# Attention and two MLPs on one core: auxiliary rows behind the next head's load, the last head ahead of the sums, additions on GpSimd moved, x divided in place

## What is computed

```python
def _attn_ref(q, k, v, s):                       # 4 batches x 8 heads, 576 tokens, 64 wide
    scores = scale * np.matmul(q, k.transpose(0, 1, 3, 2))
    cum = np.cumsum(np.maximum(s, 0.0), axis=-1)
    bias = -(cum[:, :, :, None] - cum[:, :, None, :])
    scores = np.where(causal, -1000000000.0, scores + np.minimum(bias, 0.0))
    attn = np.exp(scores - np.max(scores, axis=-1, keepdims=True))
    attn = attn / (np.sum(attn, axis=-1, keepdims=True) + 1e-09)
    return np.matmul(attn, v)

def _moe_ref(x, w_in, w_out, g_ln):              # 2304 tokens, 512 -> 1024 -> 512
    h = x @ w_in
    e = np.exp(h - np.max(h, axis=-1, keepdims=True))
    solu = h * (e / (np.sum(e, axis=-1, keepdims=True) + 1e-09))
    ln = (solu - mean(solu)) / np.sqrt(var(solu) + 1e-06) * g_ln
    return ln @ w_out

def _moe2_ref(x, w1, w2, w3, w_out):             # 512 -> 768 -> 512
    return np.maximum(np.maximum(x @ w1, x @ w2), x @ w3) @ w_out
```

## Time and profile before

| what | value |
|---|---|
| median of three runs | 773.01 us (772.12, 773.01, 778.3) |
| the profiled execution | 773.02 us, span 771.2 us |
| TensorE matmuls | 722.3 us busy, 94% of the span |
| VectorE | 394.9 us, 51% |
| ScalarE | 327.0 us, 42% |
| GpSimd | 251.4 us, 33% |
| DMA | 59.42 MB, mean 77 GB/s |

### The profile page before, as it was taken

How to read it: one execution, slowest core, us unless ns; L and a number is a source line. 1 busy time by engine, 2 the same in 40 slices (tenths; PEclk the granted TensorE clock), 3 DMA queues, 4 the chain that set the end, 5 groups by cost and what they waited for, 6 DMA issues and landing times.

```text
span 771.2 us, 12703 instructions
## 1 busy us (share of the span) xinstructions
PE 722.3 (94%) x4248; PEld 664.4 (86%) x4248; DVE 394.9 (51%) x702; ACT 327.0 (42%) x795; POOL 251.4 (33%) x248
## 2 busy tenths in 40 slices
PE   2799999999878899999999999999999999999997
PEld 2788888888767688989898989999989999899995
DVE  8898988888853675636354364612203213132120
ACT  1798888898853443424233242412112112121111
POOL 6766779888872842606040200000000000000000
PEclk9999999999998999999999999999999999999999
DMA  6598887878765312306100031000010000100101
GB/s 142 114 215 195 198 184 181 186 185 190 160 146 113 84 35 48 82 1 170 36 0 0 0 106 59 1 14 28 1 42 1 13 29 1 38 2 0 41 0 41
DMA packets 58227, 59.42 MB, mean 77 GB/s; under 512 B 23572, under 2 KB 45204, under 8 KB 58164
## 3 DMA queue, kind: packets, MB, share of 16 engines
q1 hardware_dynamic: 58196, 59.02, 32.0%
HBM read 44.15 MB, written 10.10 MB: 70 GB/s over the span
## 4 chain that ended last, share of the span: by engine, by line
PE 71%; DVE 8%; issue 6%; POOL 5%; DMA 4%; ACT 3%; SPq 2%; DVEq 0%; POOLq 0%; ACTq 0%
PE ps L652 10%; PE ps L653 10%; PE ps L651 10%; PE ps L584 4%; PE ps L586 4%; PE ps L585 4%; DMA qk_raw<-in_qk_dram 4%; PE ps L572 3%; PE ps L574 3%; PE ps L573 3%; PE ps L664 3%; PE ps L665 3%; PE ps L666 3%; PE ps L481 3%; DVE lnT_lo L1170 1%
## 5 line engine op out<-in xcount | busy, mean ns | idle before, releaser
L653 PE MATMUL ps<-x_lo,w_hi 128*128 (+1 forms) x432 | 144.4, 334 | 0.0
L651 PE MATMUL ps<-x_hi,w_hi 128*128 128x384 f32 x432 | 144.4, 334 | 0.0
L652 PE MATMUL ps<-x_hi,w_lo 128*128 128x384 f32 x432 | 144.4, 334 | 0.0
L481 PE MATMUL ps<-ident,probs 128*128 128x128 f32 x480 | 78.2, 289 | 21.9 <-DVE pt_lo L1069 15.6
L844 ACT ACTIVATE probs<-ps,nmax 128x576 f32<-128x576 f32 (+4 forms) x160 | 83.0, 539 | 17.7 <-DVE nmax L1062 17.5
L1069 DVE TENSOR_TENSOR pt_lo<-ps,pt_hi 128x512 fp32r<-128x512 f32 (+1 forms) x128 | 78.3, 652 | 11.6 <-ACT pt_hi L854 8.3
L481 PEld LDWEIGHTS ps<-ident,probs 128*128 128x128 f32 x480 | 52.4, 144 | 33.9 <-DVE pt_lo L1069 21.7
L651 PEld LDWEIGHTS ps<-x_hi,w_hi 128*128 128x128 f32 x432 | 81.1, 188 | 0.2
L652 PEld LDWEIGHTS ps<-x_hi,w_lo 128*128 128x128 f32 x432 | 81.1, 188 | 0.2
L653 PEld LDWEIGHTS ps<-x_lo,w_hi 128*128 128x128 f32 x432 | 81.1, 188 | 0.0
L854 ACT ACTIVATE pt_hi<-ps 128x512 fp32r<-128x512 f32 (+1 forms) x128 | 69.9, 572 | 26.4 <-PE ps L481 22.6
(11 more groups left out here) (101 smaller groups left out, 1436.3 us busy)
## 6 DMA issues: line engine op xcount, KB each, us to landing
qk_raw<-in_qk_dram SPq DMA_DIRECT2D x64, 288.0 KB, 4.4
xT<-halves SPq DMA_DIRECT2D x32, 144.0 KB, 2.5
xb_dram<-halves SPq DMA_DIRECT2D x32, 144.0 KB, 2.4
xb<-xb_dram SPq DMA_DIRECT2D x24, 192.0 KB, 3.9
rinvB<-rsum_dram SPq DMA_DIRECT2D x24, 192.0 KB, 4.1
stage<-in_moe_w_dram SPq DMA_DIRECT2D x18, 256.0 KB, 4.3
out_dram<-stage SPq DMA_DIRECT2D x18, 256.0 KB, 2.0
v_raw<-in_v_dram SPq DMA_DIRECT2D x32, 128.0 KB, 4.1
```

Source lines behind the costliest of these rows:

```text
L481: mm = pe.transpose(ps[:, GBANK[g], P * n:P * (n + 1)], probs[1 - par][:, o:o + P], ident[:, :])
L651: pe.matmul(dst, w_hi[f][:, i, c, :], x2_hi[par][:, c, :], start=(c == 0), stop=False)
L652: pe.matmul(dst, w_lo[f][:, i, c, :], x2_hi[par][:, c, :], start=False, stop=False)
L653: mm = pe.matmul(dst, w_hi[f][:, i, c, :], x2_lo[:, c, bass.ds(g * GT, GT)], start=False, stop=(c == KC - 1))
```

## The change

1. `reload(t)` loads q and k of head t, the values of head t-2, and then the auxiliary rows of head t-1 (not t), for which it waits for the scores of head t-3.
2. Head 31 is loaded before `store_rinv`. Its auxiliary rows come behind `store_rinv`, and the loads and stores behind these have another order.
3. On GpSimd `join(0)` goes behind the split of head 31 and of head 29's values, and `divide(0)` directly behind it, ahead of the split of head 30's values. `join(1)` stays between the values of heads 30 and 31.
4. `rinvB` has two buffers, and `divide` writes into `xT`; `xg` is gone. `divide(g)` no longer waits for `x_lo_ready`. `load_rinv(g)` is issued one group earlier.

```diff
+            def reload_aux(t, par):
+                sp.wait_ge(scores_done, 3 * (t - 1))
+                load_aux(t, par)
...
                 load_qk(t, par)
                 if known is None or known >= 4:
                     reload_v(t - 2, par)
-                if known == 2:
+                if known == 3:
                     sp.wait_ge(aux_stored, 16)
-                sp.wait_ge(scores_done, 3 * (t - 1))
-                load_aux(t, par)
+                if known is None or known >= 3:
+                    reload_aux(t - 1, 1 - par)
                 if known is None or known >= 5:
                     store_x(t - 5, 1 - par)
...
             reload(HEADS - 2, 0)
+            reload(HEADS - 1, 1)
             sp.wait_ge(rinv_done, 1)
             store_rinv(slice(0, LAST))
-            reload(HEADS - 1, 1)
+            reload_aux(HEADS - 1, 1)
+            reload_v(HEADS - 2, 0)
+            store_x(HEADS - 5, 1)
             sp.wait_ge(rinv_stored, 16 * NCH)
             load_rinv(0)
-            load_xb(1)
-            reload_v(HEADS - 2, 0)
-            store_x(HEADS - 5, 1)
             reload_v(HEADS - 1, 1)
             store_x(HEADS - 4, 0)
+            load_rinv(1)
+            load_xb(1)
             store_x(HEADS - 3, 1)
+            store_x(HEADS - 2, 0)
             load_xb(2)
             sp.wait_ge(xg_ready, 1)
-            load_rinv(1)
-            store_x(HEADS - 2, 0)
+            load_rinv(2)
             store_x(HEADS - 1, 1)
...
-            for g in range(2, NG):
-                sp.wait_ge(xg_ready, g)
+            for g in range(3, NG):
+                load_xb(g)
+                sp.wait_ge(xg_ready, g - 1)
                 load_rinv(g)
-                if g + 1 < NG:
-                    load_xb(g + 1)
...
-            def divide(g, known):
+            def divide(g, par):
                 cols = xT[:, :, bass.ds(g * GT, GT)]
-                pool.wait_ge(rinvB_loaded, 64 * (g + 1))
-                if known != 0:
-                    pool.wait_ge(x_lo_ready, 3 * g)
+                pool.wait_ge(rinvB_loaded[par], (g - par) * 32 + 64)
                 pool.wait_ge(x_added, g + 1)
-                pool.tensor_tensor(xg[:, :, :], cols, rinvB[:, :, :], ALU.mult).then_inc(xg_ready, 1)
+                pool.tensor_tensor(cols, cols, rinvB[par][:, :, :], ALU.mult).then_inc(xg_ready, 1)
...
+            slot(HEADS - 2, 0, HEADS - 2)
             join(0)
-            slot(HEADS - 2, 0, HEADS - 2)
+            divide(0, 0)
             slot(HEADS - 1, 1, HEADS - 1)
             join(1)
-            divide(0, 0)
             slot(HEADS, 0, HEADS)
-            divide(1, None)
+            divide(1, 1)
             join(2)
```

More of the change, by code:

```diff
@@ L111, in attention_and_mlp @@
         ab_.__enter__()
-        rinvB = sb(ab_, "rinvB", [P, KC, GT])
-        xg = sb(ab_, "xg", [P, KC, GT])
+        rinvB = [sb(ab_, f"rinvB{i}", [P, KC, GT]) for i in range(2)]
         xb = sb(ab_, "xb", [P, KC, GT])
@@ L220, in attention_and_mlp @@
         wout_lo_ready = sem("wout_lo_ready")
-        rinvB_loaded = sem("rinvB_loaded")
+        rinvB_loaded = [sem(f"rinvB_loaded{i}") for i in range(2)]
         xg_ready = sem("xg_ready")
@@ L393, in load_rinv @@
                         src = rsum_dram[HB * b_:HB * (b_ + 1), s0:s0 + GT // 2].rearrange("(j r) t -> r j t", r=2)[par:par + 1]
-                        dst = rinvB[D * par:D * (par + 1), :, part * GT // 2:(part + 1) * GT // 2]
-                        sp.dma_start(dst, src.broadcast_to([D, KC, GT // 2])).then_inc(rinvB_loaded, 16)
+                        dst = rinvB[g % 2][D * par:D * (par + 1), :, part * GT // 2:(part + 1) * GT // 2]
+                        sp.dma_start(dst, src.broadcast_to([D, KC, GT // 2])).then_inc(rinvB_loaded[g % 2], 16)
             LAST = HEADS - HB
@@ L811, in group @@
                 if more and not first:
-                    divide(g + 1, None)
+                    divide(g + 1, 1 - base)
                 for i in range(3):
@@ L911, in x_high @@
                     act.wait_ge(h_done, 3 * g + i - 1)
-                act.activation(x_hi[ab][:, :, :], xg[:, :, P * i:P * (i + 1)], ACT.Copy).then_inc(x_hi_ready, 1)
+                act.activation(x_hi[ab][:, :, :], xT[:, :, bass.ds(g * GT + P * i, P)], ACT.Copy).then_inc(x_hi_ready, 1)
             def gate(g, i, ab, first):
@@ L1122, in x_low @@
                 dve.wait_ge(x_hi_ready, 3 * g + i + 1)
-                dve.tensor_tensor(x_lo[ab][:, :, :], xg[:, :, P * i:P * (i + 1)], f32(x_hi[ab][:, :, :]),
+                dve.tensor_tensor(x_lo[ab][:, :, :], xT[:, :, bass.ds(g * GT + P * i, P)], f32(x_hi[ab][:, :, :]),
                                   ALU.subtract).then_inc(x_lo_ready, 1)
```

## The result

The changed kernel takes 767.65 us (median of 7 runs, 766.3 to 770.56) beside 773.47 us (7 runs) of the kernel before on the same chip: a ratio of 0.9925, with an interval of 0.9897 to 0.9952. That is 5.8 us less, where 12.6 were forecast (760.4, range 756 to 767). The kernel is faster, but by less than 1%, and lies 0.65 us outside the range. The profiled execution took 766.3 us, with a span of 764.5 us; that of before had 771.2, so the two traces differ by 6.7 us.

What follows compares the result with a forecast made beforehand. TensorE was taken as the bound, so only its waits and slow clock could give time back. Terms 3.4 + 0.9 + 4.2 + 3.6 + 0.5 = 12.6 us took 773.0 to 760.4 us, range 756 to 767.

Steps and rivals of the forecast that it cites:

- Part 1: Slots 3 to 27: auxiliary rows behind the next head's load let qk_raw come earlier; 3.4 us net of charges.
- one of the two places named: SP's next stop after L301: the store of the outputs (x_copied) or the split of the previous head; no separate size.
- 4.5 - 0.5: Slots 3 to 26: 4.5 us from earlier loads, less 0.5 for PE waiting on later auxiliary rows.
- the 0.5 charged: Slots other than 27: cost of auxiliary rows landing late for PE, 0.5 us; slot 27 had its own 0.6.
- the 5.6 us: Slots 3 to 26: their excess over undisturbed slots of 6.21 us, taken as the upper bound of the gain.
- Part 2: Slots 28 and 30: earlier loads, with join(0) later on GpSimd, win 0.9 us and 4.2 us.
- Part 3: Slot 32 to the first hidden matmul: GpSimd's reordered additions and divisions win 3.6 us; in-place division 0.
- The clock's term: First hidden matmul and its neighbours: 0.5 us added because they no longer run at the low clock.
- A: Early slots and slot 28 gain nothing because DMA engines keep loads late: 764.7; 0.21 jointly with the GpSimd rival.
- B: Seam: divide(0) or join(1) delays a split_v 2 us beyond cover, clock falls: 764.4; 0.21 jointly with the DMA rival.
- the forecast's own case: Whole kernel: the expected outcome, 757.5 to 762.5 us, given a chance of 0.56.

Runs made afterwards that it cites:

- all three versions: Versions where divide(2) has no wait for x_low: the changed kernel, 767.65 us; the kernel before with in-place division, 782.66; the fastest version without the wait, 766.05.

## Why the prediction was right and wrong

**Part 1, the auxiliary rows.** Right in its mechanism, 1.0 us too high. SP waits at L300 no more; it waits for the copied outputs (L341, 29.2 us in 23 pieces), one of the two places named. Slots 3 to 26 gained 3.0 us, where 4.5 - 0.5 were put. The waits for the rows in them were 0.46, 0.17 and 0.49, 1.1 against the 0.5 charged, but the slots with them (6, 8 and 10) are together only 0.4 us over the normal 6.21 each. More is left where the prediction put nothing: slots 17, 21 and 25 still wait 0.35 us each for `pt_lo` and take 6.68 us, 1.4 too much together. So 4.5 of the 5.6 us was too much to expect. Slot 27 waited 1.11 us and became 0.5 longer, against 0.6.

The Trainium skill, DMA: Bandwidth & Descriptors, Queues, rings and completion order, was cited for the small load not landing ahead of the `v` load. The two versions with the order turned round are consistent with it: with `v` issued first PE waited 0.17 to 0.49 us in early slots, with the rows first not at all. They don't prove it, since the rows are then also issued about 1.2 us earlier. And in slot 27 the `v` loads were not what counted: with the rows ahead of them the wait was still 1.03 us.

**Part 2, slots 28 and 30.** Right: 1.0 for 0.9, and 4.25 for 4.2. The two runs that take one half away show that, with the rest of the change, neither half does it alone.

**Part 3, the seam.** Right in size (3.7 for 3.6), and in that GpSimd blocks no `v_hl`: PE has no wait for it. The path was somewhat other. GpSimd's rows there:

```profile
216.58 3.49 POOL L781 TENSOR_TENSOR xT<-xT,rinvB 128x1536 f32<-128x1536 f32 x1 [1.94 <-DMA rinvB<-rsum_dram]
...
225.88 3.50 POOL L774 TENSOR_TENSOR xT<-xT,xb 128x1536 f32<-128x1536 f32 x1 [4.99 <-DMA xb<-xb_dram]
```

`divide(0)` waited 1.94 us for `rinvB` and ended at 220.07, 2.9 us earlier than the 223.0 worked out, as all of the seam stands 2.9 us earlier than put there (slot 31 starts at 214.58, not 217.45: the prediction held slots 3 to 26 unchanged on that scale). Relative to slot 31 it ends 5.5 us after its start, as forecast.

**The step that failed** is the last of Part 3: "Dividing in place removes no instruction; it lets `divide(g+1)` go before `x_low` has read the old tile. PE doesn't wait for `xg` after 250 us, so it is worth 0, with bounds of 1 us either way for VectorE's and GpSimd's shared use of memory." Its first half is true. But it asked only who waits for the division, and not what the division runs beside once nothing holds it back. It measures a loss of 5.5 us (5.6 to 6.3 in the stage) against 0 with bounds of 1. Rows of before for such a collision were there and not used (they are shown above): `wout_lo` with a longest of 1535 ns against a median of 742 and `normalize` with 2.94 us, where it takes 1.20 elsewhere. They show that the two engines delay each other: there it is 0.8 us of delay under an instruction whose own length is 1.2, and the division's own length is 3.5. A bound of 0.55 + 3.5 = 4 us for one held instruction could have been read there instead of 1. Nor was the engine behind it followed: `wout_low`, `lnT_lo` and PE stand in one chain, and a wait of PE of over 3 us can cost clock as well, as the earlier trace rows had shown for slot 32; behind this one the clock fell in all three versions.

**The clock's term** of 0.5 us was right in kind (the first hidden matmul takes 0.47 instead of 0.73 us) but the same mechanism took 2.4 us behind the new wait at 264.

**The rivals.** A and B (764.7 and 764.4) lie nearer to the measured 767.65 than the forecast does, but neither happened: loads were early, and GpSimd blocked no `split_v`. With the wait put back the time is 762.2 us, inside the range that was given for the forecast's own case (757.5 to 762.5). Against the kernel before in the same series (773.34) that is 11.1 of the 12.6 us. In the profiled executions the stages up to the next `turn_ln` give 0.25 + 11.7 + 0.5 = 12.5 us, and 1.5 go off again in the rest. So the sum was right there, with small errors that cancel: slots 3 to 26 gave 0.7 us less than put (151.34 us), the start, slots 27 and 28 and the seam a little more. That it comes out so close is in part luck.

## What to carry to other kernels

A wait that looks needless may be what keeps two engines apart. Before removing one, list what the freed instruction will run beside: here VectorE's instructions with two SBUF inputs stood still until GpSimd's had ended. Then follow the held engine's queue to PE; if PE waits at its end, the clock may be lost too. When a load moves in a queue, cost the small transfers behind it, since here PE waited for them and not for the moved load. And before a difference of 1 or 2 us between two medians is booked to an edit, compare the stages that it does not touch.
